# A fused attention and two-layer feed-forward kernel: the first matrix of each layer by seven block products

## The reference

```python
scores = scale * np.matmul(q_c, k_c.transpose(0, 1, 2, 4, 3))
scores = scores - np.max(scores, axis=-1, keepdims=True)
attn = np.exp(scores)
attn = attn / (np.sum(attn, axis=-1, keepdims=True) + 1e-09)
out = np.matmul(attn, v_c)
...
h = x @ w_in                                        # layer one, 512 -> 2048
g = np.maximum(h, 0.0) + alpha * np.minimum(h, 0.0)
y = g @ w_out                                       # 2048 -> 512
...
h = y @ w_in2                                       # layer two
g = h - np.tanh(h)
out = g @ w_out2
```

## Time and profile before

| | us |
|---|---|
| median of 3 runs | 1715.79 (1713.49 to 1717.57) |
| the profiled execution, its own time | 1714.71 |
| its span | 1712.8 |
| TensorE busy | 1665.1 |
| VectorE busy | 709.3 |
| ScalarE busy | 397.3 |
| GpSimd busy | 77.6 |

### The profile page before, as it was taken

The page is one execution under the profiler, slowest core; times in us unless marked ns, Lnnn a source line. Parts: engine busy times, 40 slices in busy tenths (PEclk is TensorE's granted clock), DMA queues, the critical chain, the costliest instruction groups (busy, mean ns, idle before and its releaser), DMA issues.

```text
span 1712.8 us, 23756 instructions
## 1 busy us (share of the span) xinstructions
PE 1665.1 (97%) x9744; PEld 1373.4 (80%) x9744; DVE 709.3 (41%) x1092; ACT 397.3 (23%) x661; POOL 77.6 (5%) x38
## 2 busy tenths in 40 slices
PE   5899999999999999999999999999999999999999
PEld 4898777777777777777788888888888888888887
DVE  5664454455545445454463323232323232323222
ACT  3321111121112111111133222222222222222222
POOL 4400000000000000000043000000000000000000
PEclk9999999999999999999999999999999999999999
DMA  4411101110110111010223000000000000000000
GB/s 172 154 38 63 38 19 63 38 62 19 62 38 20 61 38 62 19 62 20 76 97 123 25 25 25 25 25 25 24 24 24 24 24 24 24 24 1 14 12 25
DMA packets 26863, 74.60 MB, mean 44 GB/s; under 512 B 3104, under 2 KB 3104, under 8 KB 25632
## 3 DMA queue, kind: packets, MB, share of 16 engines
q1 hardware_dynamic: 26784, 73.42, 12.0%
HBM read 54.53 MB, written 18.87 MB: 43 GB/s over the span
## 4 chain that ended last, share of the span: by engine, by line
PE 88%; DVE 7%; issue 2%; ACT 1%; DMA 1%; SPq 0%; DVEq 0%
PE h_bank L369 14%; PE h_bank L371 14%; PE h_bank L370 14%; PE y_bank L395 8%; PE y_bank L397 8%; PE y_bank L396 8%; PE y_bank L390 7%; PE y_bank L392 6%; PE y_bank L391 6%; DVE probs L593 1%; DVE g_part L629 1%; DVE row_sum L587 1%; PE a_bank L332 1%; DVE g_full L631 1%; PE a_bank L317 1%
## 5 line engine op out<-in xcount | busy, mean ns | idle before, releaser
L369 PE MATMUL h_bank<-x_hi,w_hi 128*128 128x512 f32 (+1 forms) x1216 | 465.1, 382 | 1.5 <-ACT x_hi L456 1.5
L370 PE MATMUL h_bank<-x_lo,w_hi 128*128 128x512 f32 (+1 forms) x1216 | 461.3, 379 | 0.0
L371 PE MATMUL h_bank<-x_hi,w_lo 128*128 128x512 f32 (+1 forms) x1216 | 461.2, 379 | 0.0
L503 ACT CAST g_hi<-g_full 128x512 fp32r<-128x512 f32 (+1 forms) x304 | 181.8, 598 | 669.1 <-DVE g_full L631 556.3
L641 DVE TENSOR_TENSOR g_lo<-g_full,g_hi 128x512 fp32r<-128x512 f32 (+1 forms) x304 | 211.2, 695 | 204.0 <-ACT g_hi L503 204.0
L635 DVE TENSOR_TENSOR g_full<-h_bank,g_part 128x512 f32<-128x512 f32 x144 | 99.6, 692 | 454.6 <-ACT g_part L492 454.6
L369 PEld LDWEIGHTS h_bank<-x_hi,w_hi 128*128 128x128 f32 x1216 | 230.3, 189 | 44.1 <-ACT x_hi L456 1.6
L371 PEld LDWEIGHTS h_bank<-x_hi,w_lo 128*128 128x128 f32 x1216 | 230.0, 189 | 42.7
L370 PEld LDWEIGHTS h_bank<-x_lo,w_hi 128*128 128x128 f32 x1216 | 230.4, 189 | 41.6
L390 PE MATMUL y_bank<-g_hi,w_hi 128*128 128x512 f32 (+1 forms) x640 | 243.8, 381 | 0.0
L629 DVE TENSOR_SCALAR g_part<-h_bank,alpha_sb 128x512 f32<-128x512 f32 (+1 forms) x160 | 111.5, 697 | 303.3 <-PE h_bank L371 302.7
(11 more groups left out here) (42 smaller groups left out, 762.6 us busy)
## 6 DMA issues: line engine op xcount, KB each, us to landing
qkv<-in_chunks SPq DMA_DIRECT2D x72, 384.0 KB, 3.4
w_stage<-in_weights SPq DMA_DIRECT2D x32, 512.0 KB, 4.5
y_between_blocks<-w_stage SPq DMA_DIRECT2D x36, 256.0 KB, 3.9
qkv<-y_between_blocks SPq DMA_DIRECT2D x9, 1024.0 KB, 4.8
out<-w_stage SPq DMA_DIRECT2D x36, 256.0 KB, 2.1
alpha_sb<-in_alpha SPq DMA_DIRECT2D x1, 8.0 KB, 8.0
```

Source lines behind the costliest of these rows:

```text
L369: nc.tensor.matmul(h, hi, x_hi[:, par, k, cols], start=k == 0, stop=False)
L370: nc.tensor.matmul(h, hi, x_lo[:, par, k, cols], start=False, stop=False)
L371: last = nc.tensor.matmul(h, lo, x_hi[:, par, k, cols], start=False, stop=k == KT - 1)
L503: nc.scalar.copy(g_hi[:, par, place], g_full[:, 0:width]).then_inc(ghi_ready, 1)
```

## The change

Tokens are taken in 6 supertiles of 768 (two halves of 384), each of which runs through layer one, then each through layer two: 12 runs (s). The first matrix of a layer is computed as a 2 x 2 block product with seven products in place of eight (Strassen's scheme in Winograd's form). The blocks of the weights are the two halves of the 512 inputs by hidden slices p and p + 8 (a pair, PAIRS = 8 of them); the blocks of the tokens' side are the halves of the inputs by the halves of the tokens. A product (numbered 1 to 7) has 2 x 3 matmuls of 384 columns. Products 6, 7, 4 accumulate in one bank, 5 and 3 in a second, 1 and 2 in a third; pairs alternate between two such sets. Between them ScalarE copies product 1 to SBUF (copy_s1), and VectorE makes u2 = s1 + bank, u3 = s1 + bank, and the blocks c22, c21 and c12 (five sums of 384 columns). The activation runs on 384 columns from the bank (act_c11) and on 1152 from SBUF (act_rest on ScalarE, activate on VectorE). All activations of a supertile are kept (g_full).

The tokens' side needs seven operands a supertile (B11, B21, T1, T3, T2, B22, T4; four are differences, x_sum_of on VectorE), each of 768 columns, split by high_x (ScalarE) and low_x (VectorE). Phase A makes the products of all pairs; phase B is the second matrix: 32 units of 12 matmuls of 384 columns in layer one (second_product), 16 units of 18 matmuls of 512 columns in layer two (token_product). Its operands go through three slots (high_g, low_g, 768 columns each). Products 4 and 3 of the last pair follow unit 0 of phase B. Attention of the next supertile runs in phase B of layer one, six units (UPS), one every five steps, with scores at age 0, normalize at age 1, transposes at age 3 and outputs at age 4 (copy_x at age 4 too). The six units of the first supertile run ahead of everything, on three pairs of banks.

Weights no longer stay in SBUF. The first supertile of each layer makes them: GpSimd forms four sums a pair (weight_sums) and the low parts, ScalarE the high parts (high_parts, ten blocks ahead), 256 columns at a time, into a ring of four groups of four blocks, and SyncE stores each group (1 MB) in DRAM. The other ten supertiles stream the 22 groups of the layer from there. Raw weights come in chunks of two DMAs of 256 KB in two buffers.

The diff, cut to its core. The first phase_a and phase_b are TensorE's, the second ScalarE's, the third VectorE's:

```diff
-TILE = 512
...
+HALF = 384
+SUPER = TOKENS // (2 * HALF)
+RUNS = 2 * SUPER
+PAIRS = FT // 2
+BLOCKS, PER_GROUP, RING = 88, 4, 4
+GROUPS = BLOCKS // PER_GROUP
+AHEAD = 10
...
+INPUT_OF = {1: B11, 2: B21, 3: B22, 4: T4, 5: T1, 6: T2, 7: T3}
+WEIGHT_OF = {1: "A11", 2: "A12", 3: "S4", 4: "A22", 5: "S1", 6: "S2", 7: "S3"}
+BANK_OF = {1: 0, 2: 0, 4: 1, 6: 1, 7: 1, 3: 2, 5: 2}
...
+def base(p):
+    return 5 + 7 * (p - 1)
+def product_at(layer, i, p):
+    if i == 4:
+        return base(p + 1) + 2 if p < PAIRS - 1 else 55 + layer
+    if i == 3:
+        return base(p + 1) + 4 if p < PAIRS - 1 else 56 + layer
+    if p == 0:
+        return {1: 0, 5: 1, 6: 2, 2: 3, 7: 4}[i]
+    return base(p) + {6: 0, 1: 1, 5: 3, 2: 5, 7: 6}[i]
...
+                nc.gpsimd.tensor_tensor(sums[:, 1, :], a11, a21, ALU.subtract).then_inc(w_sum, 1)
+                pool.wait_ge(w_sum, first + 1)
+                nc.gpsimd.tensor_tensor(a21, a21, a22, ALU.add).then_inc(w_sum, 1)
+                pool.wait_ge(w_sum, first + 2)
+                nc.gpsimd.tensor_tensor(sums[:, 0, :], a21, a11, ALU.subtract).then_inc(w_sum, 1)
+                pool.wait_ge(w_sum, first + 3)
+                nc.gpsimd.tensor_tensor(sums[:, 2 + p % 2, :], a12, sums[:, 0, :], ALU.subtract).then_inc(w_sum, 1)
...
+            for s in range(0, RUNS, SUPER):
+                for j in range(BLOCKS):
+                    what, i, p = block_use(layer_of(s), j)
+                    if what == "product" and i == (6 if p else 1):
+                        weight_sums(s, j, p)
+                    low_part(s, j)
...
+            def product(s, i, p):
+                j = product_at(layer_of(s), i, p)
+                weights_ready(s, j)
+                if i in (1, 5, 6):
+                    bank_free(s, i, p)
+                elif i == 2:
+                    pe.wait_ge(s1_ready, after_pairs(s, p))
+                elif i == 7:
+                    pe.wait_ge(u2_ready, after_pairs(s, p))
+                elif i == 4:
+                    pe.wait_ge(u3_ready, after_pairs(s, p))
+                else:
+                    pe.wait_ge(c22_ready, after_pairs(s, p))
...
+                for k in range(2):
+                    hi, lo = w[:, 0, k * P:(k + 1) * P], w[:, 1, k * P:(k + 1) * P]
+                    nc.tensor.matmul(h, hi, xo_hi[:, o, k, :], start=fresh and k == 0, stop=False, skip_group_check=not fresh)
+                    nc.tensor.matmul(h, hi, xo_lo[:, o, k, :], start=False, stop=False, skip_group_check=not fresh)
+                    last = nc.tensor.matmul(h, lo, xo_hi[:, o, k, :], start=False, stop=k == 1, skip_group_check=not fresh)
+                last.then_inc(block_done, 1)
...
+            def phase_a(s):
+                product(s, 1, 0)
+                product(s, 5, 0)
+                product(s, 6, 0)
+                product(s, 2, 0)
+                product(s, 7, 0)
+                for p in range(1, PAIRS):
+                    product(s, 6, p)
+                    product(s, 1, p)
+                    product(s, 4, p - 1)
+                    product(s, 5, p)
+                    product(s, 3, p - 1)
+                    product(s, 2, p)
+                    product(s, 7, p)
+            def phase_b(s):
+                for n in range(units_in(layer_of(s))):
+                    if layer_of(s) == 0:
+                        attention(s, n)
+                        second_product(s, n)
                     else:
+                        token_product(s, n)
+                    if n == 0:
+                        product(s, 4, PAIRS - 1)
+                        product(s, 3, PAIRS - 1)
...
+            def phase_a(s):
+                high_parts(s, AHEAD)
+                copy_s1(s, 0)
+                for p in range(1, PAIRS):
+                    high_parts(s, base(p) + 1 + AHEAD)
+                    copy_s1(s, p)
+                    act_c11(s, p - 1)
+                    high_parts(s, base(p) + 3 + AHEAD)
+                    act_rest(s, p - 1)
+                    high_parts(s, base(p) + 6 + AHEAD)
+                high_g(s, 0)
+                high_g(s, 1)
+                act_c11(s, PAIRS - 1)
...
+                    if n + 2 < units_in(layer):
+                        high_g(s, n + 2)
+                    if n == 0:
+                        act_rest(s, PAIRS - 1)
+                    high_parts(s, unit_at(layer, n) + AHEAD)
+                    if layer == 0:
+                        attention(s, n)
...
+            def phase_a(s):
+                for p in range(PAIRS):
+                    sum_u2(s, p)
+                    if p:
+                        activate_c11(s, p - 1)
+                        sum_c21(s, p - 1)
+                        sum_c12(s, p - 1)
+                    if p == PAIRS - 1:
+                        low_g(s, 0)
+                        low_g(s, 1)
+                    sum_u3(s, p)
+                    sum_c22(s, p)
+                    if p:
+                        activate(s, p - 1)
...
+                    if n == 0:
+                        activate_c11(s, PAIRS - 1)
+                        low_g(s, 2)
+                        sum_c21(s, PAIRS - 1)
+                        sum_c12(s, PAIRS - 1)
+                        activate(s, PAIRS - 1)
+                    if layer == 0:
+                        attention(s, n)
+                    if n and n + 2 < units_in(layer):
+                        low_g(s, n + 2)
...
+                        if n == 31:
+                            x_sum_of(s + 1, T1)
+                            x_sum_of(s + 1, T3)
+                            low_x(s + 1, T1)
...
+                    read_y(s, 2)
+                    read_y(s, 3)
+                    if s < SUPER - 1:
+                        low_x(s + 1, T3)
+                        x_sum_of(s + 1, T2)
+                        low_x(s + 1, T2)
+                        low_x(s + 1, B22)
+                        x_sum_of(s + 1, T4)
+                        low_x(s + 1, T4)
...
+                if c >= 2:
+                    sp.wait_ge(wlo_ready, made_index(s, raw_uses(layer)[c - 2]) + 1)
...
+                before, last = group_last(s, q * PER_GROUP)
+                sp.wait_ge(block_done, done(before, last))
+                if made_here(before):
+                    sp.wait_ge(w_stored[group % RING], 16 * stores_of(before, last))
+                if s == made + 1:
+                    sp.wait_ge(w_stored[(made * GROUPS + q) % RING], 16 * stores_of(made, q * PER_GROUP))
+                sp.dma_start(ring[:, group % RING, :, :, :].rearrange("x b h n -> x (b h n)").bitcast(F32),
+                             w_dram[layer_of(s), q, :, :]).then_inc(ring_in[group % RING], 16)
...
```

More of the change, by code:

```diff
@@ L58, in due @@
-def due(n, slot, stage, behind=0):
-    period, at = (OPEN_PERIOD, OPEN_STAGE_AT) if is_first(n) else (PERIOD, STAGE_AT)
-    c, rest = divmod(slot - behind - at[stage], period)
-    if rest or not 0 <= c < (2 * UPT - OPEN_UNITS if is_first(n) else UPT):
-        return None
-    return divmod(OPEN_UNITS + c, UPT) if is_first(n) else (n + 1, c)
-def is_first(n):
-    return isinstance(n, int) and n == 0
-def has_attention(n, layer):
-    return layer == 0 and not (isinstance(n, int) and n == TILES - 1)
```

1138 lines of the change are left out of this document (710 added, 428 removed).

## The result

The changed kernel takes 1784.12 us (median, 1783.33 to 1789.18); the kernel before, run beside it, 1715.12 (1713.49 to 1717.57). The ratio is 1.0407, interval 1.0384 to 1.0431: slower by 69 us, where the prediction said slower by 24 and put 1778 at the end of its range. The profiled execution has a span of 1782.5 us against 1712.8.

What follows compares the result with a forecast made beforehand. TensorE, busy 97% of the span, was taken to bound the kernel before. Products of 1489.8 us plus opening, attention, turns, weight making, transfers and tail gave 1729.0, with clock 1737 of span, 1740 us forecast; range 1694 to 1778.

Steps and rivals of the forecast that it cites:

- the gain of 82 us in products: All TensorE products: 1489.8 us in place of 1572.1, a gain of 82.3, with 384-column matmuls at 0.1733 us.
- Part 5: Turn from phase B to A: TensorE waits for operands, 26.8 us over five turns in layer one, nothing in layer two.
- Part 4: Turn from phase A to B: TensorE waits behind activations and splits, 41.9 us in layer one, 15.3 in layer two.
- The opening: Start of the kernel: six attention units and the first operands run before products, costing 48.8 us, bounds 40 and 55.
- Part 8: TensorE's clock: gaps of 2 to 4 us at 17 turns may halve it, taken as 8 us, bounds 0 and 42.
- Rival C: TensorE's clock: every turn drops it, 17 x 2.4 = 41 us in place of 8, total 1773; chance 0.10.
- Part 6: The two weight-making supertiles: GpSimd's period of 10.4 us a pair exceeds TensorE's 7.28, costing 28 us, bounds 0 and 45.
- Rival A: Weight making: GpSimd's period fits at about 7.3 us, so its stalls and the clock loss vanish, total 1700; chance 0.28.
- Rival B: Weight making: GpSimd also waits for VectorE on the shared port, period 12.3 us, total 1765; chance 0.10.
- Part 7: DMA transfers: streamed groups hidden, output stores beside blocks, late loads of attention units 6 us, bounds 0 and 15.
- Part 3: Attention in phase B: thirty units at 2.3 us without the wait for normalize, 69 us, bounds 61 and 92.

Runs made afterwards that it cites:

- step4: The changed kernel with attention units every four steps of phase B instead of five, and operands T1, T3, T2, B22, T4 made in steps 26 to 30: 1759.07 us.
- fillall: The changed kernel with filler matmuls on ready data, into an unused bank, at every long TensorE pause of supertiles 2 to 5: 1774.18 us, ratio 1.0344.
- combo3: The changed kernel with earlier g splits, four-step attention, third raw buffer, late x load, output stores first, later operands for the seventh supertile: 1696.43 us, ratio 0.9889.
- outfirst: The changed kernel with only the issue of layer two's output stores moved ahead of the load of the next group: 1775.93 us, ratio 1.0358.

## Why the prediction was right and wrong

**Right.** The direction, and for the reason given: the gain of 82 us in products is there (the 384-column spacing, read off a line between two neighbours, held within 0.8 ns), and the rest grew by more. Part 5: 26.8 against 21.0, and step4 took it away. Part 4 in layer one: 41.9 against 42.3, from 3.0 and 4.1 a turn; the first wait measured 2.74, and the 4.1 put down to unit 3 were two waits, 2.13 for the bank of act_c11 and 2.33 at unit 3, so that the sum is in part luck. In layer two the turn cost 1.69, and the 0.65 for a bank did not show. The opening, 48.8 against 48.4, is luck in part too: the forecast holds 2.5 us of half clock that the measured row does not, and the first product came at 41.47, not near 39. Attention with its loads, parts 3 and 7: 75 against 75.1.

**Part 8, the clock, was 21 of the 45 us.** The step that failed was to set the turns' waits one at a time beside the earlier trace rows, a fall at an idle time of 5.56 and none at 1.90, and to take 8 us, the price of three or four falls, for gaps that lay between the two. The price of a fall, 2.3 us, was about right; the number was not. There were 14: one in the opening, five in the weight-making supertiles, five at the turns B to A, two at turns A to B and one behind a wait for a unit load. fillall shows that the pauses are the cause. How long they are counts: in the last five supertiles of the changed kernel and the twelve others, where pauses stand alone, none of the 63 of 1.56 to 1.97 us (between starts) was followed by a fall, 10 of the 17 of 1.99 to 3.05 were, and all five of 3.66 to 3.99. That they come in groups seems to count too: the turn B to A, with 2.41 and mostly 1.8 us and 0.95 between them, was followed by a fall in all 30 cases (six kernels that keep it), the three pauses of the turn A to B, within 17 us, in 19 of 30. No run has the 2.41 alone at that place, so this is not shown. Rival C (17 turns of 2.4, 41 us) was nearer than the forecast, but too high; its "every turn" did not hold: the turns in layer two, single pauses of 1.69, cost nothing. The Trainium skill (TensorE: Matmul & The Clock Gate, section HAM oscillation — how this bites in real kernels) tells of a DMA wait in every tile of a loop that sends the clock down in every tile; the trace agrees for layer one, with 2.1 to 2.6 us lost after each of its five turns B to A, and not for layer two.

**Part 6, weight making: 28 against 43.6.** The period was about right, 10.4 against 9.2 to 11.4 in the first supertile. The step that failed came after it: seven pairs of 10.4 - 7.28 are 22 us, less three blocks of slack (3.1) is 19, and the text took 9 for the first supertile and 1.5 for its turn; it measured 19.5 (33.6 us of pauses, less 6.9 of the opening and 7.2 of a usual turn), 14.2 of it within phase A. In the seventh, the x load in front of a raw chunk (part 7 says nothing of it) made one pause of 8.3, and at its turn a raw chunk, asked for behind group stores that wait for low parts, another of 8. Rival A (the period fits) is out. Rival B was half right: combo3 shows GpSimd stretched to 1.33 beside VectorE, so its period stays near 10 us even with no wait for a chunk, by coincidence what the late chunk had made of it. The Trainium skill (SBUF — State Buffer, section Who interferes with whom) has the port pair locked for a whole instruction whichever engine comes first; the trace agrees in both directions, 1.33 for GpSimd's 0.74 here, and VectorE's 2.37 for 0.43 in the earlier trace rows.

**Part 7, transfers.** "Stores of outputs lie beside blocks" cost 9.2 us. The ring was costed for bandwidth and cover, rightly, and it never starved. The late one was a store in the same queue, whose buffer is written again by sum_c22 of pair 0. The 6 us for unit loads were there and larger: six waits of the scores, 10.9 us.

**Part 3 and the sixth supertile.** A unit took some 2.1 us without the waits for its load, 2.3 in the forecast. The operands of the first supertile of layer two, "nothing" in part 5, cost 3.3: they share steps of 2.08 us with low_g there, and steps twice as long in layer two.

**What stays open.** Where the clock falls among several pauses is not settled: outfirst has the same turns in layer one as the changed kernel, yet its clock fell also near 447 and 460 us, where the changed kernel's did not. Of the 19.5 us of pauses in the first supertile of combo3, the 11.5 behind the opening were not tried, nor were its waits of the scores for copy_x.

## What to carry to other kernels

Price the pauses of TensorE beyond their length. Here two of 2.41 and 1.8 us close together cost some 2.5 more in clock each time, single ones of 2 to 3 us cost it in 10 of 17 cases, and those under 2 cost nothing. Mending one pause may only move it to the next wait, or make a longer one of two. When an operation becomes cheaper on the busy engine, lay out each turn's queue orders on the other engines, as this paid best here: the changed kernel lost 4% and, with those orders mended, the same arithmetic gained 1.1%. For each DMA ask not only what bandwidth it takes but what stands behind it in its queue, and which buffer is written next when it lands.

## What the runs showed of the hardware beyond what was expected

- Pauses of 1.7 to 2.9 us, none as long as the 5.56 of the earlier trace rows, hold the mean granted clock of layer one at 0.97; without them it is 1.00.
- The first 384-column step behind a group of attention matmuls takes 0.26 to 0.28 us to the next start in place of 0.17, at a granted clock of 1.00: 83 times, 8.6 us in the changed kernel.
- A 256-column operation of GpSimd takes 0.72 to 0.74 us alone and 1.33 to 1.44 beside VectorE; the floor of part 6, a quarter of the 1024-column one (0.60), was too low.
- Six 256 KB stores land in 2.1 us (median) when they are issued ahead of a 1 MB load, in 6.6 behind it; a pair of 256 KB chunks behind a 1.5 MB load lands after some 9 us.
